# Issuing the weighted products of two attention units one behind the other

## The reference

```python
scores = scale * np.matmul(q, k.transpose(0, 1, 3, 2))
mask = (rel >= 0) & (rel < 64)
scores = np.where(mask, scores, -1000000000.0)
scores = scores - np.max(scores, axis=-1, keepdims=True)
attn = np.exp(scores)
attn = attn / (np.sum(attn, axis=-1, keepdims=True) + 1e-09)
return np.matmul(attn, v)
```

## Time and profile before

| | |
|---|---|
| median of 3 runs | 810.62 us (810.16 to 811.32) |
| the profiled execution | 810.14 us, its span 808.2 us |
| PE busy | 799.2 us (99%) |
| DVE, ACT, POOL busy | 488.0 (60%), 305.8 (38%), 205.3 us (25%) |
| granted PE clock | 0.998 of full speed |
| chain that ended last | PE 96% |

### The profile page before, as it was taken

The page is one execution under the profiler, slowest core; times in us unless marked ns, Lnnn a source line. Parts: engine busy times, 40 slices in busy tenths (PEclk is TensorE's granted clock), DMA queues, the critical chain, the costliest instruction groups (busy, mean ns, idle before and its releaser), DMA issues.

```text
span 808.2 us, 14997 instructions
## 1 busy us (share of the span) xinstructions
PE 799.2 (99%) x4797; PEld 719.6 (89%) x4798; DVE 488.0 (60%) x993; ACT 305.8 (38%) x667; POOL 205.3 (25%) x187
## 2 busy tenths in 40 slices
PE   9999999999999999999999999999999999999996
PEld 8999999999999999999999999988888888888885
DVE  7989645667657764857586667736226445564352
ACT  7989743121321132121213123435324534543341
POOL 5565995040004000500130000051920110110100
PEclk9999999999999999999999999999999999999999
DMA  7998950020002002000200013326353643755100
GB/s 223 303 316 285 339 228 1 1 78 1 1 1 79 0 1 75 6 1 1 79 0 1 1 40 105 111 77 217 136 187 131 249 155 130 258 188 199 55 15 26
DMA packets 42720, 86.88 MB, mean 107 GB/s; under 512 B 6494, under 2 KB 16990, under 8 KB 42144
## 3 DMA queue, kind: packets, MB, share of 16 engines
q1 hardware_dynamic: 36144, 75.41, 26.8%
q0 software_dynamic: 3360, 10.40, 3.8%
q10 hardware_dynamic: 3152, 0.26, 0.3%
HBM read 72.54 MB, written 14.30 MB: 107 GB/s over the span
## 4 chain that ended last, share of the span: by engine, by line
PE 96%; DMA 1%; issue 1%; DVE 1%; ACT 1%; SPq 0%; ACTq 0%; POOLq 0%; DVEq 0%
PE ps L1126 28%; PE ps L1128 28%; PE ps L1127 28%; PE ps L1059 3%; PE ps L1275 2%; PE ps L1094 2%; PE ps L1079 1%; PE ps L1193 1%; DMA kt<-kT 1%; PE ps L1053 1%; ACT pr L795 0%; PE ps L1035 0%; DMA out<-osb,sidx 0%; PE ps L1303 0%; DVE nmax L1430 0%
## 5 line engine op out<-in xcount | busy, mean ns | idle before, releaser
L1126 PE MATMUL ps<-xn_hi,GV_hi 128*128 128x384 f32 x576 | 194.2, 337 | 0.0
L1128 PE MATMUL ps<-xn_hi,GV_lo 128*128 128x384 f32 x576 | 193.4, 336 | 0.0
L1127 PE MATMUL ps<-xn_lo,GV_hi 128*128 128x384 f32 x576 | 192.9, 335 | 0.0
L1126 PEld LDWEIGHTS ps<-xn_hi,GV_hi 128*128 128x128 f32 x576 | 108.2, 188 | 2.8
L1127 PEld LDWEIGHTS ps<-xn_lo,GV_hi 128*128 128x128 f32 x576 | 108.2, 188 | 2.7
L1128 PEld LDWEIGHTS ps<-xn_hi,GV_lo 128*128 128x128 f32 x576 | 108.1, 188 | 0.0
L853 ACT ACTIVATE h_hi<-ps 128x384 fp32r<-128x384 f32 x72 | 35.5, 493 | 160.8 <-DVE ps L1520 159.0
L1550 DVE CUSTOM_DVE_ANT_0 ps<-ysb,wrb 128x512 f32<-128x512 f32 x120 | 92.2, 769 | 6.0 <-ACT ysb L860 1.0
L847 ACT ACTIVATE sig<-ps 128x384 f32<-128x384 f32 x71 | 35.0, 493 | 159.9 <-PE ps L1128 140.7
L1128 PE MATMUL ps<-Wo_hi,h_lo 128*128 128x512 f32 x216 | 85.5, 396 | 0.0
L1127 PE MATMUL ps<-Wo_lo,h_hi 128*128 128x512 f32 x216 | 85.3, 395 | 0.0
(11 more groups left out here) (185 smaller groups left out, 1363.3 us busy)
## 6 DMA issues: line engine op xcount, KB each, us to landing
EW_raw<-w SPq DMA_DIRECT2D x32, 1024.0 KB, 7.6
vt<-vW SPq DMA_DIRECT2D x16, 512.0 KB, 5.2
y_rows<-ysb SPq DMA_DIRECT2D x6, 768.0 KB, 3.9
kt<-kT SPq DMA_DIRECT2D x47, 96.0 KB, 4.6
qraw<-qT SPq DMA_DIRECT2D x15, 288.0 KB, 4.1
xraw<-xT_rows SPq DMA_DIRECT2D x5, 768.0 KB, 5.4
xT_rows<-xo SPq DMA_DIRECT2D x12, 288.0 KB, 3.5
raw_out<-w_out SPq DMA_DIRECT2D x3, 1024.0 KB, 7.9
```

The lines of the kernel that those rows point to most:

```text
L1126: nc.tensor.matmul(out, a_hi, b_hi, start=start, stop=False)
L1127: nc.tensor.matmul(out, a_hi, b_lo, start=False, stop=False)
L1128: return nc.tensor.matmul(out, a_lo, b_hi, start=False, stop=stop)
```

## The change

The weighted products move. For units 0 to 11 those of units 2p - 2 and 2p - 1 are issued together, in step 0 of the odd unit 2p + 1 (pair p = 1 to 6); the last pair of the loop (units 14 and 15) is taken out of it and keeps one product in each unit. For this `pt` gets a second buffer; the results of a pair lie behind one another in banks 5, 6 and 7 (the second begins at column 576); the reciprocals of step 1 move from bank 7 to the score bank of step 1, and the scores of step 1 wait for the multiplication three steps back instead of the exponentials. ACT copies both results in the odd unit, one behind the exponentials of step 1 and one behind those of step 2, both after both products. `copy_pt` and `move_pt` wait for the product two units back. SP's order is rewritten by pairs. At the end of attention the first mean squares move behind the product of unit 14 and one transpose.

```diff
-        pt = r.take("pt", JOBS, BPJ * P)
+        pt = [r.take(f"pt{u}", JOBS, BPJ * P) for u in range(2)]
...
+            def queries_keys(n, u, q=True, between=None):
+
                 if q:
                     load_q(n + 3, 1 - u)
...
+                load_k(n + 2, u, 0)
+                if between is not None:
+                    between()
+                load_keys(n + 2, u, range(1, JOBS))
+
+            def store_of(n):
+                return store_rest if n < PAIRS else store_xT
+
+            for pair in range(1, UNITS // 2 - 1):
+                n = 2 * pair
+                if pair > 1:
+                    queries_keys(n, 0, True, lambda: store_of(n - 4)(n - 4, 0))
+                    store_of(n - 3)(n - 3, 1)
+                else:
+                    queries_keys(n, 0)
+                if pair <= KEPT:
+                    load_half(pair - 1, 0)
+                else:
+                    load_quarter(pair - KEPT - 1, 0)
+                queries_keys(n + 1, 1, pair < UNITS // 2 - 2, lambda: load_v(n, 0))
+                load_v(n + 1, 1)
+                if pair <= KEPT:
+                    load_half(pair - 1, 1)
+                else:
+                    load_quarter(pair - KEPT - 1, 1)
+            store_xT(UNITS - 6, 0)
+            load_v(UNITS - 2, 0)
+            store_xT(UNITS - 5, 1)
+            load_v(UNITS - 1, 1)
+            store_xT(UNITS - 4, 0)
+            store_xT(UNITS - 3, 1)
...
             def move_pt(n, u):
 
                 act.wait_ge(pt_ready, done(JOBS * n + JOBS))
-                act.wait_ge(o_ready, done(n))
-                nc.scalar.activation(pt[:, JOBS - 1, :], ps[:, T_BANK + (JOBS * u + JOBS - 1) % 2, 0:BPJ * P],
+                act.wait_ge(o_ready, done(n - 1))
+                nc.scalar.activation(pt[u][:, JOBS - 1, :], ps[:, T_BANK + (JOBS * u + JOBS - 1) % 2, 0:BPJ * P],
                                      ACT.Copy).then_inc(pt_moved, 1)
 
-            def copy_o(n, u, stored, kept=False):
-
-                act.wait_ge(o_ready, done(n + 1))
+            def copy_o(n, u, stored, kept=False, ahead=0):
+
+                act.wait_ge(o_ready, done(n + 1 + ahead))
                 act.wait_ge(xT_out[u], stored)
-                o = ps[:, O_BANK:O_BANK + 2, :].rearrange("p a c -> p (a c)")
+                o = ps[:, O_BANK:O_BANK + 3, :].rearrange("p a c -> p (a c)")[:, u * S:(u + 1) * S]
...
-                    if b == 0:
-                        copy_o(2 * pair + u - O_LAG, u, 16 * pair, kept)
+                    if closing and (u, b) in ((0, 1), (1, 0)):
+                        copy_o(2 * pair - O_LAG + u, u, 16 * pair)
+                    elif not closing and u == 1 and b > 0:
+                        n = 2 * pair - O_LAG + b - 1
+                        copy_o(n, b - 1, 16 * pair, isinstance(pair, int) and n < PAIRS, 2 - b)
...
                 pe.wait_ge(k_in[u][b], loads)
-                pe.wait_ge(exp_ready, done(j - 2))
+                pe.wait_ge(p_ready if b == 1 else exp_ready, done(j - 2))
...
-            def weighted(n, u, loads):
+            def weighted(n, u, loads, paired=False):
...
-                pe.wait_ge(o_copied, done(n))
+                pe.wait_ge(o_copied, done(n - 1 if paired else n))
                 for k in range(NBLK):
-                    bank, at = O_BANK + k * WIN // BANK, k * WIN % BANK
+                    bank, at = O_BANK + (u * S + k * WIN) // BANK, (u * S + k * WIN) % BANK
...
-                    if b == 0:
+                    if b == 0 and closing:
                         weighted(n - O_LAG, u, 16 * pair)
-
-            with pe.Fori(1, UNITS // 2) as pair:
+                    elif b == 0 and u == 1:
+                        weighted(2 * pair - O_LAG, 0, 16 * pair)
+                        weighted(2 * pair - O_LAG + 1, 1, 16 * pair, True)
+
+            with pe.Fori(1, UNITS // 2 - 1) as pair:
                 pair_of_units(pair)
+            pair_of_units(UNITS // 2 - 1, True)
...
                 pe.wait_ge(exp_ready, done(STEPS - 1))
-                first_mean_squares()
                 weights_T(UNITS - 1, 1, 0)
                 half_gate(c, 0, par, *gv_weights[0], range(1, 2))
                 weighted(UNITS - 2, 0, 8 * UNITS)
                 weights_T(UNITS - 1, 1, 1)
+                first_mean_squares()
...
                 if b == 1:
-                    bank = MISC
+                    bank = S_BANK + b
...
             def copy_pt(n, u, b):
                 dve.wait_ge(pt_ready, done(JOBS * n + b + 1))
-                dve.wait_ge(o_ready, done(n))
-                nc.vector.tensor_copy(pt[:, b, :], ps[:, T_BANK + (JOBS * u + b) % 2, 0:BPJ * P]).then_inc(pt_copied, 1)
+                dve.wait_ge(o_ready, done(n - 1))
+                nc.vector.tensor_copy(pt[u][:, b, :], ps[:, T_BANK + (JOBS * u + b) % 2, 0:BPJ * P]).then_inc(pt_copied, 1)
```

More of the change, by code:

```diff
@@ L453, in _ @@
             load_keys(3, 1)
-            def unit(n, u, q=True, k=True, half=None, quarter=None, store=store_xT):
-                store(n - 2, u)
+            def queries_keys(n, u, q=True, between=None):
                 if q:
                     load_q(n + 3, 1 - u)
[L459 to L478, removed]
+                load_k(n + 2, u, 0)
[27 more added lines that the diff above has]
+            store_xT(UNITS - 3, 1)
             load_wo(0)
@@ L820, in _, with pair_of_units @@
                 exps(j, u, b)
-            def pair_of_units(pair, kept=False):
+            def pair_of_units(pair, closing=False):
                 for j, u, b in jobs(2 * JOBS * pair, 2 * JOBS):
@@ L832, in _ @@
             for pair in range(1, KEPT + 1):
-                pair_of_units(pair, True)
-            with act.Fori(KEPT + 1, UNITS // 2) as pair:
                 pair_of_units(pair)
+            with act.Fori(KEPT + 1, UNITS // 2 - 1) as pair:
+                pair_of_units(pair)
+            pair_of_units(UNITS // 2 - 1, True)
             def root(c, bank=MISC):
@@ L1094, in weighted @@
                         last = nc.tensor.matmul(ps[half, bank, at:at + WIN], vt[u][:, max(k - 1, 0), half],
-                                                pt[:, k // BPJ, at_k:at_k + WIN], start=True, stop=True)
+                                                pt[u][:, k // BPJ, at_k:at_k + WIN], start=True, stop=True)
                 last.then_inc(o_ready, 1)
@@ L1110, in _, with pair_of_units @@
                     weights_T(u - 1, u - 1, b)
-            def pair_of_units(pair):
+            def pair_of_units(pair, closing=False):
                 for j, u, b in jobs(2 * JOBS * pair, 2 * JOBS):
```

## The result

The changed kernel takes **818.53 us** in the median of 5 runs (816.20 to 820.28), the kernel before on the same chip 810.98 (5 runs): a ratio of 1.0088, interval 1.0075 to 1.0100. The total was right; of its terms one came out half as large, one larger, and one part of the time was not in the sum at all. The profiled execution took 818.79 us; its span, 817.0, is 8.8 above the 808.2 of before.

What follows compares the result with a forecast made beforehand. PE was taken to bound the kernel, busy 99% of the span, with a loop through ACT binding after the change. Loops, close and small terms gave +7.9, less 0.9 of waits +7.0: 817.6 us on the 810.62 median, range 814.5 to 820.0.

Steps and rivals of the forecast that it cites:

- What binds: In attention: PE fills all 9.56 us of a pair, with DVE (8.81) and ACT (8.93) nearly full too.
- Rival A: In attention: PE stays the limit, ACT and DVE run ahead enough, six double products save 1.4 us; 809.0; chance 4%.
- D: Closing pair: the loop binds, but the wait there is covered; 815, counted within the main case's 86%.
- Part 1: Two weighted products in a row, six pairs: 2.26 us (bounds 2.10 and 2.40), saving PE 0.2 per pair, 1.4 in six.
- Part 2: Units 3 to 13: a loop through ACT once per pair takes 10.59 us against 9.56; five loops, +5.4.
- Rival B: In attention's pairs: DVE's loop binds, ACT's doesn't; 9.87 us, +0.3 per pair; 811.6, no change; chance 5%.
- Part 3: Closing pair: unit 14's product waits for the twelfth copy, 5.83 us instead of 3.57, +2.3; the next product +0.5.
- The second product's +0.48: Closing pair: the next product waits 4.05 us for unit 13's move, which stands behind a copy.
- Rival C: Closing pair: PE's 2.3 us wait before unit 14's product might lower the clock for a unit; +4, 821.6; chance 5%.
- Part 4: Second buffer, SP's order, query layout and moved mean squares are free; only a 0.1 us PE wait goes.
- The sum: Whole kernel: 5.39 - 0.10 + 2.26 + 0.48 - 0.10 = +7.9 us, +7.0 once 0.9 of waits vanish.
- The irregular waits: In attention: 0.9 us of PE waits over seven pairs, expected to vanish into PE's waiting for ACT.

## Why the prediction was right, and where not

- **What binds.** Right: PE's own work went down and it waits once per pair; the loop, its order and the place of each idle are as forecast. Rival A (809.0) is out by all five windows; D (815) is out by the wait of 2.15 in the closing pair.
- **Part 1**, 2.25 against 2.26: right, between bounds of 2.10 and 2.40. The saved turn is there (2.25 where two single products take 2 x 1.20 from start to masks), and it decides nothing. The Trainium skill, "TensorEngine Tiling (Array Packing)", section "Key Properties", says that a change of tiling mode drains the engine; these rows agree.
- **Part 2**, the failing step: "copy 0.70 (0.66 and a turn); move 0.57". The rows give an instruction's length, not when the next can start; the copy in a chain costs 0.53 and the move 0.37. The loop is 0.55 longer per pair, not 1.03. The rows at hand showed it: the copy in two parts starts 29.84 and 30.21, 0.37 apart, while the first lasts 0.50. And the 0.57 read behind the move was no price of the move: the next exponential stood there for DVE's maximum, which ended at 61.97, 0.12 before it.

```profile
61.42 0.55 DVE L1430 TENSOR_REDUCE nmax<-ps 128x3 f32<-128x384 f32 x1
```

- **Rival B.** Set aside at 5% because it "needs copies that cost ACT nothing". With copies cut to a ninth the pair still takes 10.0: DVE's loop was mis-sized by the same 0.12 of transposes waiting for a multiplication, and only 0.1 lies between it and ACT's. Neither engine alone is the bound; a loop over PE, DVE and ACT is. Cutting copies would not have rescued the change. (The 811.6 named for this rival fits six pairs of +0.31 less 0.9; with the five loops it is 811.3.)
- **Part 3.** The place of the product was right (5.80 against 5.83), and the copy accounts for it. "Values have a whole pair" was wrong in the one place that mattered: there they are asked for behind unit 15's first keys, the product starts 0.43 after the copy's end, and with the copy short they still hold it for 1.7. The second product's +0.48 is not seen by itself.
- **Rival C**, 5%, came in part: the clock was granted at half behind this wait, for 3.4 us, and cost 1.6, not 4. It fell likewise behind waits of 1.87 (values early) and 1.94 (reciprocals in SBUF). Waits of 0.7 to 1.4 at the same place (four experiments) left it at 1.00, but so did 1.71 (short copies) and, one unit later, 1.88 (the last run with scores ahead), so the length of the wait alone does not decide it in these runs. The Trainium skill, "TensorE: Matmul & The Clock Gate", section "Why this matters for your kernels", warns of idle gaps between bursts of matmuls. Its gaps are longer than these: the traces agree that a gap can halve the clock, and show it behind shorter ones than the page has.
- **Part 4.** "It buys nothing" was wrong for the second buffer: alone it is worth 0.9 us (0.9989 of 810.7). DVE is not PE's limit on average, but PE's weight load had waited up to 0.2 for ACT's move into `pt` in seven units. The mean squares (nothing) were right, and the wait for step 1 too in the kernel without pairs; in the changed kernel PE stands for the multiplication 0.64 and 0.53 before the first pair, and whether the 0.35 lost there is theirs was not tried.
- **The sum.** Attention: forecast +7.0, measured +6.2 (loops 2.1 less, close 1.1 more, start 0.45 more, tail 0.3 less). The irregular waits, put at -0.9, did not all vanish: the five loops hold 51.12 - 5 x 10.11 = 0.57 of them, against 48.73 - 5 x 9.56 = 0.93 before. The collision of gather and fetch, +1.3, was in no term. That the total is off by 0.9 only is luck in part: these errors cancel.

## What to carry to other kernels

Putting two bursts of the busiest engine side by side saves a turn, here 0.2 us, and leaves its helpers without work for the length of two and then behind for the rest; trace the loop that closes over all engines, once around, before counting on the average slack. Cost an instruction inside a chain by the distance between starts of neighbours, not by its length. Where a schedule is moved, look at its last, irregular round by itself: half of this loss is there.

## What the runs showed of the hardware

- A DVE multiplication of 128x384 float32 with its second operand in SBUF takes 0.56 while POOL is quiet and up to 1.58 while POOL works, and POOL's layout of queries 2.03 instead of 1.47; with that operand (12 bytes per partition) in PSUM it stays at 0.55 throughout. The Trainium skill, "SBUF — State Buffer", section "Who interferes with whom", says that a DVE instruction with two SBUF inputs contends with a GpSimd instruction that reads SBUF; these rows agree. One tiny operand in PSUM is worth about 4 us here (818.53 against 822.43).
- Waits of 1.87 to 2.15 us in the middle of full PE work were followed by 3.4 us at 1.2 GHz in three traces, beginning 0.1 to 1.4 us after PE resumed; waits of 1.71 and 1.88 in two others were not. In the changed kernel three of five executions show the lower mean clock. Where the clock falls, the wait's own length is not its price.
- One instruction fetch of 16 KB beside two indirect gathers goes with a last packet 0.7 to 1.0 us later and a first gather that lands after 5.0 us instead of 3.3, in code that the change had not touched.
